# Windowed attention and two expert layers: the second expert's two products by Strassen's scheme

## The chip, the cores and the metric

The kernel runs on one core of one Trainium2 chip. The metric is the device time of one execution in microseconds, the median of several runs. A profiled execution was taken beside them; all rows below come from it. TensorE runs the matmuls (PE in the rows; its weight loads are PEld), VectorE is DVE, ScalarE is ACT, GpSimd is POOL, and SyncE (SP) issues most transfers; POOL issues those of the weights.

## What is computed

Comments on the right tell the sizes.

```python
def _attn_ref(q, k, v, mem_k, mem_v):          # 4 x 8 heads, 768 rows of 64
    ...
    for c in range(nc):                          # chunks of 32 rows, 16 to the left, 8 to the right, 8 memory rows
        ...
        scores = scale * np.matmul(q_c, k_full.transpose(0, 1, 3, 2))
        scores = scores - np.max(scores, axis=-1, keepdims=True)
        a = np.exp(scores)
        a = a / (np.sum(a, axis=-1, keepdims=True) + 1e-09)
        out[:, :, c_start:c_end] = np.matmul(a, v_full)

def _moe_ref(x, w_in, w_out):                    # 3072 x 512, 512 x 2048, 2048 x 512
    h = x @ w_in
    g = h * np.cos(h)
    return (g @ w_out).astype(np.float32)

def _moe2_ref(x, w1, w2, w3, w_out):             # 3072 x 512, three 512 x 768, 768 x 512
    h = np.maximum(np.maximum(x @ w1, x @ w2), x @ w3)
    return (h @ w_out).astype(np.float32)
```

All is float32. Both kernels split an operand of a large product into a rounded high part and the rest (the low part), and add three products: high by high, high by low, low by high.

## The kernel before

**Stage 1** works on eight blocks of 384 tokens (`BLK`), block t with the first expert while the attention of block t+1 is slipped in between. One step f of 16 makes 128 of the 2048 hidden columns (`hidden` on PE, 12 matmuls of 384 columns) and adds hidden column group f-3 (`second`, 12 matmuls of 384 columns) to the four banks of the result (`LAG` = 3). ACT scales and rounds the hidden values (L505, L507), DVE forms the remainder (L667), ACT takes sine and square (L514, L516), DVE multiplies and splits into `gh` and `gl` (L671, L677, L680). The result of a block goes to DRAM (`y_dram`).

**Stage 2** works on the same eight blocks. For one of six groups m of 128 hidden columns, PE makes three branches (12 matmuls of 384 columns each, `branch`), ACT copies the first from PSUM (L598), DVE takes the largest of the three (L755, L758) and splits it (L764, L766), and PE multiplies the group before by the output weights (`project`, L461 to L463, 9 matmuls of 512 columns, three banks of 128 tokens). A block is 6 x (36 + 9) matmuls.

**Weights** come in slots of 1024 columns a partition: POOL issues the load into `wraw` (two buffers), ACT rounds it (`high_w`, L535), POOL subtracts (`low_w`, L288). The ones of stage 2 take the place of stage 1's in `wts`, slot by slot, during the last block of stage 1, one a step from step 4 on: ACT's `high_w(NF + f - LAG - 1)` stands ahead of `hidden(t, f)` in its order.

**What sets the order**: no scheduler. Each engine has its own program, written by hand, and executes it strictly in that order; semaphores tie the engines together. An engine that waits holds up all that stands behind the wait in its own program. The two stages' middle blocks run in hardware loops (`Fori`).

The three lines that make every large product:

```python
pe.matmul(o, wh, mh, start=start, stop=False)          # L306
pe.matmul(o, wh, ml, start=False, stop=False)          # L307
return pe.matmul(o, wl, mh, start=False, stop=stop)    # L308
```

## Times and profile before

| | |
|---|---|
| median of 3 runs | 1063.84 us (1062.72 to 1064.02) |
| the profiled execution's own time | 1065.7 us |
| its span, first to last instruction | 1063.9 us |
| PE busy | 1028.1 us, 97% of the span |
| DVE, ACT, POOL busy | 493.2, 386.4, 83.7 us |
| stage 1 ends, by the last split of its hidden values | about 659 us |
| chain that ended last | PE 89%, ACT 4%, DVE 3%, DMA 3% |

Matmuls overlap: the 384-column ones take 0.33 us each but start every 0.173 us, so the distance between starts is what a matmul costs. A busy row is a duration; a row's last bracket tells how long the engine stood idle before it and for whom.

### The profile page before, as it was taken

To read this page: it belongs to the slowest core of one execution; us is meant where nothing else is said; L and a number is where in the kernel's file an instruction comes from. 1 tells how busy PE (TensorE), PEld (TensorE's weight loads), DVE (VectorE), ACT (ScalarE), POOL (GpSimd) and SP (SyncE) were. 2 spreads that over 40 slices of the span, in tenths; PEclk is the share of its full clock that TensorE was granted. 3 is DMA by queue.
4 is the path that set the end of the run, shared out by engine and by line. 5 is a ranking of instruction groups with operands and counts; after the bars stand their busy time and mean duration, and the time that the engine had idled before them with its cause. 6 is when DMAs were issued, how large, how long until landed. Compare 5 with 4: busy or idle time off the path is not lost.

```text
span 1063.9 us, 17509 instructions
## 1 busy us (share of the span) xinstructions
PE 1028.1 (97%) x6976; PEld 981.0 (92%) x6976; DVE 493.2 (46%) x876; ACT 386.4 (36%) x703; POOL 83.7 (8%) x64
## 2 busy tenths in 40 slices
PE   5789999999999999999999999999999999999998
PEld 4688999999999999999999988999999999999997
DVE  5477555554554555554655566323232223323222
ACT  2566454454454464464454554111010110101000
POOL 1555000000000000000000354000000000000000
PEclk7899999999999999999999999999999999999999
DMA  8754240231321321321311231201000000000000
GB/s 206 186 153 137 52 110 22 76 83 41 82 59 41 90 50 41 92 49 40 90 31 40 70 103 57 89 20 41 30 30 30 30 30 30 30 30 30 0 30 30
DMA packets 35712, 65.97 MB, mean 62 GB/s; under 512 B 2368, under 2 KB 26944, under 8 KB 35648
## 3 DMA queue, kind: packets, MB, share of 16 engines
q1 hardware_dynamic: 31616, 50.34, 17.3%
...
## 4 chain that ended last, share of the span: by engine, by line
PE 89%; ACT 4%; DVE 3%; DMA 3%; issue 2%; POOL 0%; SPq 0%; ACTq 0%; DVEq 0%
PE ps L306 25%; PE ps L308 24%; PE ps L307 24%; PE ps L462 3%; PE ps L463 3%; PE ps L461 3%; PE ps L351 2%; PE ps L325 2%; DVE stage_and_tiles L667 2%; DMA qk<-qk_in 1%; PE ps L359 1%; PE ps L338 1%; ACT wts L535 1%; DMA wraw<-w_in 1%; ACT stage_and_tiles L514 1%
## 5 line engine op out<-in xcount | busy, mean ns | idle before, releaser
L306 PE MATMUL ps<-xh,wts 128*128 128x384 f32 x1088 | 373.7, 344 | 3.5 <-issue 2.1
L308 PE MATMUL ps<-xh,wts 128*128 128x384 f32 x1088 | 365.5, 336 | 0.0
L307 PE MATMUL ps<-xl,wts 128*128 128x384 f32 x1088 | 364.7, 335 | 0.0
L306 PEld LDWEIGHTS ps<-xh,wts 128*128 128x128 f32 x1088 | 204.8, 188 | 14.9 <-issue 11.0
L667 DVE SCALAR_TENSOR_TENSOR stage_and_tiles<-stage_and_tiles 128x384 f32<-128x384 f32 x128 | 101.6, 794 | 240.5 <-ACT stage_and_tiles L507 240.5
L307 PEld LDWEIGHTS ps<-xl,wts 128*128 128x128 f32 x1088 | 205.0, 188 | 2.0
L308 PEld LDWEIGHTS ps<-xh,wts 128*128 128x128 f32 x1088 | 204.7, 188 | 0.0
L306 PE MATMUL ps<-gh,wts 128*128 128x384 f32 x512 | 171.9, 336 | 3.9 <-DVE gl L680 3.9
L308 PE MATMUL ps<-gh,wts 128*128 128x384 f32 x512 | 171.4, 335 | 0.0
L307 PE MATMUL ps<-gl,wts 128*128 128x384 f32 x512 | 171.1, 334 | 0.0
L598 ACT COPY stage_and_tiles<-ps 128x384 f32<-128x384 f32 x48 | 23.0, 479 | 306.0 <-PE ps L308 305.5
L505 ACT ACTIVATE stage_and_tiles<-ps 128x384 f32<-128x384 f32 x128 | 62.7, 490 | 162.2 <-PE ps L308 159.2
L755 DVE TENSOR_TENSOR stage_and_tiles<-stage_and_tiles,ps 128x384 f32<-128x384 f32 x48 | 26.6, 554 | 201.4 <-PE ps L308 201.4
L288 POOL TENSOR_TENSOR wts<-wraw,wts 128x1024 fp32r<-128x1024 f32 x28 | 66.8, 2384 | 550.9 <-ACT wts L535 550.9
L514 ACT ACTIVATE stage_and_tiles<-stage_and_tiles 128x384 f32<-128x384 f32 x128 | 67.2, 525 | 99.9 <-DVE stage_and_tiles L667 99.1
L306 PEld LDWEIGHTS ps<-gh,wts 128*128 128x128 f32 x512 | 96.1, 188 | 6.5 <-DVE gl L680 6.5
L307 PEld LDWEIGHTS ps<-gl,wts 128*128 128x128 f32 x512 | 96.1, 188 | 0.0
L308 PEld LDWEIGHTS ps<-gh,wts 128*128 128x128 f32 x512 | 96.1, 188 | 0.0
L680 DVE TENSOR_TENSOR gl<-stage_and_tiles,gh 128x384 fp32r<-128x384 f32 x128 | 71.5, 558 | 4.4
L507 ACT ACTIVATE stage_and_tiles<-ps,rounder 128x384 f32<-128x384 f32 x128 | 73.5, 574 | 0.0
L671 DVE SCALAR_TENSOR_TENSOR stage_and_tiles<-stage_and_tiles 128x384 f32<-128x384 f32 x128 | 70.4, 550 | 0.0
L516 ACT ACTIVATE stage_and_tiles<-stage_and_tiles 128x384 f32<-128x384 f32 x128 | 67.2, 525 | 4.0
...
## 6 DMA issues: line engine op xcount, KB each, us to landing
...
wraw<-w_in POOLq DMA_DIRECT2D x28, 512.0 KB, 3.7
...
y_dram<-stage_and_tiles SPq DMA_DIRECT2D x8, 768.0 KB, 6.5
qk<-y_dram SPq DMA_DIRECT2D x8, 768.0 KB, 4.3
out<-stage_and_tiles SPq DMA_DIRECT2D x8, 768.0 KB, 3.5
...
```

The costliest lines, as they stand in the source:

```text
L288: pool.tensor_tensor(wts[:, s, :, 1, :], wraw[:, g % 2, :, :], wts[:, s, :, 0, :].bitcast(F32), ALU.subtract).then_inc(w_ready, 1)
L306: pe.matmul(o, wh, mh, start=start, stop=False)
L307: pe.matmul(o, wh, ml, start=False, stop=False)
L308: return pe.matmul(o, wl, mh, start=False, stop=stop)
L461: pe.matmul(o, gh[:, m % 3, toks], w[:, 0, :], start=(m == 0), stop=False)
L505: act.activation(hid[:, f % 2, :], ps[:, HB[f % 2], 0:BLK], ACT.Copy, scale=1.0 / (2 * PI)).then_inc(h_copied, 1)
L507: act.activation(ang[:, f % 2, :], ps[:, HB[f % 2], 0:BLK], ACT.Identity, scale=1.0 / (2 * PI), bias=rounder[:, :]).then_inc(turns_done, 1)
L514: act.activation(a, a, ACT.Sin, scale=BELOW_PI).then_inc(sin_done, 1)
L516: act.activation(a, a, ACT.Square, scale=ROOT_TWO).then_inc(cos_done, 1)
L667: dve.scalar_tensor_tensor(out=a, in0=a, scalar=ROUND, in1=hid[:, f % 2, :], op0=ALU.subtract, op1=ALU.subtract).then_inc(r_done, 1)
L671: dve.scalar_tensor_tensor(out=hp, in0=ap, scalar=1.0, in1=hp, op0=ALU.subtract, op1=ALU.mult).then_inc(g_done, 1)
L680: dve.tensor_tensor(glp, hp, ghp.bitcast(F32), ALU.subtract).then_inc(g_ready, 1)
```

## The change

Stage 1 stays, but for the last block's extra work. **Stage 2** is done anew, on six blocks of 512 tokens (`BLK2`). A product of 2 x 2 blocks is made with seven block products in place of eight (the Winograd form of Strassen's scheme). Blocks of the input are 128 model columns by 256 tokens, blocks of the weights 128 by 128.

- A **unit** of the first product (54 of them: 6 blocks x 3 pairs of column groups x 3 branches) is seven products 1, 5, 7, 2, 6, 4, 3 of 6 matmuls with 256 columns: 42. A unit of the second product (12: 6 blocks x 2 halves) is seven products of 9 matmuls with 256 columns: 63. PE interleaves products 7 and 4 of unit n-1 with the other five of unit n. All in all 3024 matmuls of 256 columns; before there were 1728 of 384 and 432 of 512. Every product has its own wait, products 6, 3, 7 and 4 for a copy or sum of what lies in their bank, since they add onto it.
- ACT copies three banks of 256 columns a unit (`snap`, products 1, 5, 6), DVE adds four quarters (`c11`, `c12`, `c22`, `c21`) and takes the largest (`largest`, 768 columns).
- **Operands in seven forms.** Each weight unit (9 of the branches and 3 of the output weights) is loaded by POOL in two transfers, POOL makes four sums of 256 columns (`sums_rows`, `sums_columns`), ACT rounds 1792 columns (`high_w2`), POOL subtracts 1792 columns (`low_w2`). Two raw buffers. The input of each block gets four sums of 512 columns (DVE, `y_sums_of`) and seven roundings and subtractions of 512 columns (`high_y` on ACT, `y_low` on DVE).
- **The hidden values** of the second product go out to DRAM (`h2_dram`, 18 pieces, 512 KB each) and come back from the end of the first product on: SP loads, POOL sums (`sums_hidden`, 4 x 256 columns), ACT rounds (`high_h`, 1792 columns), DVE subtracts (`h_low`, 1792 columns). `H_STEPS` places the roundings in ACT's and DVE's program, from unit 50 on.
- All of stage 2 is written out without loops. Buffers are cut from three arenas (`arena_w`, `arena_a`, `arena_f`).

```diff
+HALF = 256
+BLK2 = 2 * HALF
+NBLK2 = B * S // BLK2
+NPAIR = NM // 2
+UNITS = NPAIR * NB2
+UNITS_A = NBLK2 * UNITS
+TAUS = HALF // SUB
+UNITS_ALL = UNITS_A + NBLK2 * TAUS
+HUNITS = NBLK2 * NPAIR
+UCOLS = 2 * 7 * HALF
+RAWCOLS = 7 * HALF
+RING = 9
+ORDER = (1, 5, 2, 6, 3, 7, 4)
+W_AT = {1: 0, 2: 1, 5: 2, 4: 3, 6: 4, 7: 5, 3: 6}
+W2B_AT = {1: 0, 7: 1, 2: 2, 3: 3, 5: 4, 6: 5, 4: 6}
+H_AT = {1: 0, 5: 1, 4: 2, 2: 3, 6: 4, 7: 5, 3: 6}
...
+        W2_STEPS = (5, 7, 9, 10, 12, 14)
+        H_STEPS = ((0,), (1,), (2,), (3,), (4, 5), (6,), (7, 8), (9,), (10, 11), (12,), (13, 14), (15,), (16, 17)) + ((),) * 6
...
+        BANK_A, BANK_B, BANK_C = (2, 1), (6, 7, 4), (5, 0)
...
+            for blk in range(NBLK2):
+                if blk < NBLK2 - 1:
+                    load_y(blk + 1)
+                else:
+                    load_h(0)
+                    load_h(1)
+                store_hidden2(3 * blk)
+                if blk == NBLK2 - 1:
+                    load_h(2)
+                store_hidden2(3 * blk + 1)
+                if blk == NBLK2 - 1:
+                    load_h(3)
+                store_hidden2(3 * blk + 2)
+            for r in range(4, 7):
+                load_h(r)
+            for blk in range(NBLK2):
+                for r in range(3 * blk + 7, min(3 * blk + 10, HUNITS)):
+                    load_h(r)
+                for tau in range(TAUS):
+                    store_out(TAUS * blk + tau)
...
+            def load_h(r):
+                sp.wait_ge(fours_stored[r % 2], 16 * (r // 2) + 16)
+                if r < 2:
+                    sp.wait_ge(y_ready, 7 * NBLK2)
+                elif r < 4:
+                    sp.wait_ge(w2_ready, UNITS + r)
+                else:
+                    sp.wait_ge(hm_ready, r - 3)
+                sp.dma_start(raw_h[r % 4][:, 0:4, :], h2_dram[r, :, :].rearrange("p (q c) -> p q c", q=4))\
+                  .then_inc(h_landed[r % 4], 16)
...
+            def load_w2(u):
+                if u == 0:
+                    pool.wait_ge(w_ready, NF)
+                elif u == 1:
+                    pool.wait_ge(pv_done, SUBS)
+                else:
+                    pool.wait_ge(w2_ready, u - 1)
...
+            def sums_rows(r, sums, base):
+                pool.tensor_tensor(r[:, 5, :], r[:, 0, :], r[:, 2, :], ALU.subtract).then_inc(sums, 1)
+                pool.tensor_tensor(r[:, 2, :], r[:, 2, :], r[:, 3, :], ALU.add).then_inc(sums, 1)
+                pool.wait_ge(sums, base + 2)
+                pool.tensor_tensor(r[:, 4, :], r[:, 2, :], r[:, 0, :], ALU.subtract).then_inc(sums, 1)
+                pool.wait_ge(sums, base + 3)
+                pool.tensor_tensor(r[:, 6, :], r[:, 1, :], r[:, 4, :], ALU.subtract).then_inc(sums, 1)
...
+            load_w2(0)
+            load_w2(1)
+            sums_w2(0)
+            for u in range(UNITS + NPAIR):
+                if u + 1 < UNITS + NPAIR:
+                    sums_w2(u + 1)
+                low_w2(u)
+                if u + 2 < UNITS + NPAIR:
+                    load_w2(u + 2)
+            for r in range(HUNITS):
+                pool.wait_ge(h_landed[r % 4], 16 * (r // 4) + 16)
+                sums_hidden(raw_h[r % 4], hm_sums, 4 * r)
...
+            def product6(n):
+                pe.wait_ge(s1_copied, n + 1)
+                product(n, 6, bank_b(n))
...
+            def product7(n):
+                pe.wait_ge(s6_copied, n + 1)
+                product(n, 7, bank_b(n))
+
+            def product4(n):
+                pe.wait_ge(c22_done, n + 1)
+                product(n, 4, bank_b(n))
+
+            for n in range(UNITS_ALL + 1):
+                if n < UNITS_ALL:
+                    product1(n)
+                    product5(n)
+                if n:
+                    product7(n - 1)
+                if n < UNITS_ALL:
+                    product2(n)
+                    product6(n)
+                if n:
+                    product4(n - 1)
+                if n < UNITS_ALL:
+                    product3(n)
...
+            def high_w2(u):
+                if u < UNITS:
+                    last = -(-UCOLS * (u + 1) // 2048) - 1
+                    act.wait_ge(y_done, NF * (NBLK - 1) + last + 1)
+                else:
+                    act.wait_ge(p_done[4], UNITS_A - UNITS + u - UNITS + 1)
+                act.wait_ge(w2_sums, 4 * u + 4)
+                act.copy(unit_w(u % UNITS)[:, 0, :, :], raw2[u % 2]).then_inc(w2_high, 1)
+
+            def high_h(r):
+                if r < 6:
+                    act.wait_ge(p_done[4], UNITS_A - UNITS + 3 + r + 1)
+                elif r < 8:
+                    act.wait_ge(p_done[4], UNITS_A)
+                else:
+                    act.wait_ge(p_done[4], UNITS_A + TAUS * ((r - 8) // NPAIR + 1))
+                act.wait_ge(hm_sums, 4 * r + 4)
+                act.copy(unit_h(r)[:, 0, :, :], raw_h[r % 4]).then_inc(hm_high, 1)
...
+                    if last and f in W2_STEPS:
+                        high_w2(W2_STEPS.index(f))
+                    if last and f in (11, 13, 15):
+                        high_y(0, (f - 11) // 2)
...
+            def snap(n, p, bank, s, spent, copied):
+                act.wait_ge(p_done[p], n + 1)
+                if n >= 2:
+                    act.wait_ge(spent, n - 1)
+                act.copy(snaps[:, n % 2, s, :], bank).then_inc(copied, 1)
...
+            for n in range(UNITS_ALL + 1):
+                blk, u = divmod(n, UNITS)
+                if n < UNITS_ALL:
+                    snap(n, 1, bank_b(n), 0, c11_done, s1_copied)
+                    snap(n, 5, bank_c(n), 1, c22_done, s5_copied)
+                if n < 3:
+                    high_w2(6 + n)
+                if n < UNITS_A:
+                    if blk < NBLK2 - 1 and u == 6:
+                        high_y(blk + 1, 0)
+                        high_y(blk + 1, 1)
+                    if blk < NBLK2 - 1 and u == 8:
+                        high_y(blk + 1, 2)
+                        high_y(blk + 1, 3)
+                    if blk and u == 0:
+                        high_y(blk, 4)
+                        high_y(blk, 5)
+                if n < UNITS_ALL:
+                    snap(n, 6, bank_b(n), 2, c12_done, s6_copied)
+                if blk and u == 0 and n < UNITS_A:
+                    high_y(blk, 6)
+                if n and (n > UNITS_A or (n - 1) % NB2 == 0):
+                    corner(n - 1)
+                if UNITS_A - 7 <= n < UNITS_A - 4:
+                    high_w2(UNITS + n - UNITS_A + 7)
+                if UNITS_A - 4 <= n:
+                    done = H_STEPS[n - UNITS_A + 4]
+                    for r in done:
+                        high_h(r)
...
+            def h_low(r):
+                dve.wait_ge(hm_high, r + 1)
+                dve.tensor_tensor(unit_h(r)[:, 1, :, :], raw_h[r % 4], unit_h(r)[:, 0, :, :].bitcast(F32),
+                                  ALU.subtract).then_inc(hm_ready, 1)
...
+            def c22(n):
+                dve.wait_ge(p_done[7], n + 1)
+                dve.wait_ge(s5_copied, n + 1)
+                dve.tensor_tensor(place(n, 2), snaps[:, n % 2, 1, :], bank_b(n), ALU.add).then_inc(c22_done, 1)
...
+            for n in range(UNITS_ALL + 1):
+                blk, u = divmod(n, UNITS)
+                before = n - 1
+                if n:
+                    c22(before)
+                    if before < UNITS_A and before % NB2:
+                        largest(before)
+                if blk and u == 0 and n < UNITS_A:
+                    y_low(blk, 4)
+                if n < UNITS_ALL:
+                    c11(n)
+                if n and before < UNITS_A and before % NB2:
+                    c21(before)
+                if blk and u == 0 and n < UNITS_A:
+                    y_low(blk, 5)
+                    y_low(blk, 6)
+                if n < UNITS_ALL:
+                    c12(n)
+                if n < UNITS_A:
+                    if blk < NBLK2 - 1 and u == 5:
+                        y_sums_of(blk + 1)
+                    if blk < NBLK2 - 1 and u == 6:
+                        y_low(blk + 1, 0)
+                        y_low(blk + 1, 1)
+                    if blk < NBLK2 - 1 and u == 8:
+                        y_low(blk + 1, 2)
+                        y_low(blk + 1, 3)
+                if UNITS_A - 4 <= n:
+                    for r in H_STEPS[n - UNITS_A + 4]:
+                        h_low(r)
```

**PE, in the middle of stage 2.** Before, the end of a `project` and the begin of a branch:

```order
L461 MATMUL ps<-wts,gh 128x512
L462 MATMUL ps<-wts,gh 128x512
L463 MATMUL ps<-wts,gl 128x512
L306 MATMUL ps<-xh,wts 128x384 [waits third_maxed]
L307 MATMUL ps<-xl,wts 128x384
L308 MATMUL ps<-xh,wts 128x384
```

After, the end of product 2 and the first half of product 6 of one unit:

```order
L474 MATMUL ps<-arena_a,arena_w 128x256
L472 MATMUL ps<-arena_a,arena_w 128x256 [waits s1_copied]
L473 MATMUL ps<-arena_a,arena_w 128x256
L474 MATMUL ps<-arena_a,arena_w 128x256
L472 MATMUL ps<-arena_a,arena_w 128x256
```

A wait stands ahead of every 6 matmuls (of 12 before), on ACT or DVE each time.

**POOL, the weights of stage 2.** Before, from one slot to the next:

```order
L288 TENSOR_TENSOR wts<-wraw,wts 128x2x512 [waits w_high]
L283 DMA wraw<-w_in 128x1024 [waits w_ready]
L288 TENSOR_TENSOR wts<-wraw,wts 128x2x512 [waits w_high]
L283 DMA wraw<-w_in 128x1024 [waits w_ready]
L288 TENSOR_TENSOR wts<-wraw,wts 128x2x512 [waits w_high]
```

After, from one unit to the next, and where the hidden values' sums begin:

```order
L451 TENSOR_TENSOR arena_w<-arena_f,arena_w 128x1792 [waits w2_high]
L416 DMA arena_f<-w_in 128x512 [waits w2_ready]
L416 DMA arena_f<-w_in 128x512
L429 TENSOR_TENSOR arena_f<-arena_f 128x256 [waits raw2_landed1]
L431 TENSOR_TENSOR arena_f<-arena_f 128x256 [waits w2_sums]
L432 TENSOR_TENSOR arena_f<-arena_f 128x256
L434 TENSOR_TENSOR arena_f<-arena_f 128x256 [waits w2_sums]
L451 TENSOR_TENSOR arena_w<-arena_f,arena_w 128x1792 [waits w2_high] x2
L437 TENSOR_TENSOR arena_f<-arena_f 128x256 [waits h_landed0]
```

The load of unit u+2 stands behind the subtraction of unit u, and its sums, which wait for the landing, stand ahead of the subtraction of unit u+1.

**ACT, units 49 to 51 of stage 2.** Before, the groups of the last block of stage 2:

```order
L598 COPY stage_and_tiles<-ps 128x384 [waits m_ready,br_done]
L581 COPY stage_and_tiles<-ps 128x512 [waits out_stored,o_done]
L581 COPY stage_and_tiles<-ps 128x512
L598 COPY stage_and_tiles<-ps 128x384 [waits m_ready,br_done] x5
L581 COPY stage_and_tiles<-ps 128x512 [waits out_stored,o_done]
```

After:

```order
L803 COPY arena_f<-ps 128x256 [waits c12_done,p6_done]
L812 COPY arena_f<-ps 128x256 [waits fours_stored0,p4_done]
L739 CAST arena_w<-arena_f 128x1792 [waits w2_sums,p4_done]
L803 COPY arena_f<-ps 128x256 [waits c11_done,p1_done]
L803 COPY arena_f<-ps 128x256 [waits c22_done,p5_done]
L803 COPY arena_f<-ps 128x256 [waits c12_done,p6_done]
L749 CAST arena_w<-arena_f 128x1792 [waits hm_sums,p4_done]
L803 COPY arena_f<-ps 128x256 [waits c11_done,p1_done]
```

The copy that product 6 of unit 51 waits for (last row) now stands behind two roundings that wait for POOL's sums.

## Rows read from the trace of the kernel before

**Rows 1.** The page's part 1: busy time, share of the span, instructions.

```profile
PE 1028.1 (97%) x6976; PEld 981.0 (92%) x6976; DVE 493.2 (46%) x876; ACT 386.4 (36%) x703; POOL 83.7 (8%) x64
```

**Rows 2.** Timeline of PE in stage 2: start us, us, engine, line, operation.

```profile
762.21 0.33 PE L308 MATMUL ps<-xh,wts 128*128 128x384 f32 x1
762.38 0.39 PE L461 MATMUL ps<-wts,gh 128*128 128x512 f32 x1
762.61 0.40 PE L462 MATMUL ps<-wts,gh 128*128 128x512 f32 x1
762.84 0.40 PE L463 MATMUL ps<-wts,gl 128*128 128x512 f32 x1
763.08 0.39 PE L461 MATMUL ps<-wts,gh 128*128 128x512 f32 x1
```

**Rows 3.** Timeline of ACT: the same group's copy, six groups apart.

```profile
674.95 0.48 ACT L598 COPY stage_and_tiles<-ps 128x384 f32<-128x384 f32 x1 [7.87 <-PE ps L308]
...
725.03 0.48 ACT L598 COPY stage_and_tiles<-ps 128x384 f32<-128x384 f32 x1 [7.87 <-PE ps L308]
```

**Rows 4.** Timeline of weight loads and matmuls, from four transposes back to `hidden`.

```profile
240.73 0.60 PE L338 MATMUL ps<-ident,prob 128*128 128x128 f32 x4
241.06 0.19 PEld L306 LDWEIGHTS ps<-xh,wts 128*128 128x128 f32 x1
241.08 0.42 PE L306 MATMUL ps<-xh,wts 128*128 128x384 f32 x1
241.17 0.19 PEld L307 LDWEIGHTS ps<-xl,wts 128*128 128x128 f32 x1
```

**Rows 5.** Timeline of POOL in the last block of stage 1.

```profile
602.49 2.40 POOL L288 TENSOR_TENSOR wts<-wraw,wts 128x1024 fp32r<-128x1024 f32 x1 [1.69 <-ACT wts L535]
605.18 0.57 POOL L283 DMA_DIRECT2D wraw<-w_in  x1 [0.30 <-POOL wts L288]
```

**Rows 6.** The page's part 6: KB each, us from issue to landing.

```profile
wraw<-w_in POOLq DMA_DIRECT2D x28, 512.0 KB, 3.7
qk<-y_dram SPq DMA_DIRECT2D x8, 768.0 KB, 4.3
```

**Rows 7.** Groups by line and shape: count, busy us, mean ns of one, idle before.

```profile
L535 ACT CAST wts<-wraw 128x1024 fp32r<-128x1024 f32 x28 | 29.0, 1034 | 1.9 <-DMA wraw<-w_in 1.9
L526 ACT CAST xh<-qk 128x1536 fp32r<-128x1536 f32 x8 | 11.9, 1482 | 0.0
L581 ACT COPY stage_and_tiles<-ps 128x512 f32<-128x512 f32 x16 | 8.6, 590 | 48.2 <-PE ps L463 48.2
L758 DVE TENSOR_TENSOR stage_and_tiles<-stage_and_tiles,ps 128x384 f32<-128x384 f32 x48 | 26.6, 554 | 71.1 <-PE ps L308 71.1
```

**Rows 8.** Timeline of ACT in the last block of stage 1, its step 3.

```profile
593.84 0.49 ACT L505 ACTIVATE stage_and_tiles<-ps 128x384 f32<-128x384 f32 x1 [0.73 <-PE ps L308]
594.23 0.57 ACT L507 ACTIVATE stage_and_tiles<-ps,rounder 128x384 f32<-128x384 f32 x1
```

**Rows 9.** DVE: L667's durations (smallest/median/largest, ns); L690's group as in Rows 7.

```profile
L667 DVE SCALAR_TENSOR_TENSOR stage_and_tiles<-stage_and_tiles x128: 495/558/2016, 39.5 to 654.5; 128x384 f32<-128x384 f32 x128
L690 DVE TENSOR_TENSOR xl<-qk,xh 128x1536 fp32r<-128x1536 f32 x8 | 15.0, 1869 | 2.0 <-ACT xh L526 2.0
```

**Rows 10.** Stretches at the start: busy time of each engine, PEclk the granted clock.

```profile
5.50:9.00 3.50, 0.00 (x0) 0.00 (x0) 1.82 (x2) 0.00 (x0) 0.00 (x0) 0.90 1.05 234
9.00:15.70 6.70, 4.77 (x68) 3.73 (x68) 2.36 (x5) 0.63 (x1) 0.52 (x1) 0.50 1.11 226
34.00:38.00 4.00, 3.71 (x12) 3.70 (x12) 0.24 (x1) 1.51 (x2) 3.13 (x3) 0.50 0.23 46
38.00:42.00 4.00, 4.00 (x47) 3.34 (x46) 2.37 (x3) 3.40 (x6) 2.76 (x2) 0.87 0.57 161
42.00:47.00 5.00, 2.16 (x13) 1.84 (x11) 3.21 (x4) 2.92 (x6) 2.93 (x2) 1.00 0.97 248
```

**Rows 11.** Timeline of ACT at the end of the kernel.

```profile
1058.83 1.07 ACT L581 COPY stage_and_tiles<-ps 128x512 f32<-128x512 f32 x2 [7.80 <-PE ps L463]
```

461 lines of the change are left out of this document (274 added, 187 removed).

## The prediction, made before the change was run

> **What bounds the kernel now.** I read part 1 first: PE is busy 97% of the span [rows 1], so a gain has to come from fewer or shorter matmuls, and every wait of PE costs its full length. Next the timeline of PE in stage 2 [rows 2]: matmuls follow each other without a gap, 0.17 us from start to start at 384 columns, 0.70 us for three at 512. ACT's copy of the same group comes back 50.08 us later after one block [rows 3], which is 216 matmuls of 384 and 54 of 512 columns. With 0.2333 us for a 512 (0.70 / 3), a 384 takes (50.08 - 54 x 0.2333) / 216 = 0.1735 us. Eight blocks are 400.6 us. PE's last matmul ends at 1058.8 [rows 11], so stage 2 has an equivalent start at 1058.8 - 400.6 = 658.2 us. I compare the new kernel with this number: its equivalent start plus its matmuls plus its waits.
>
> **Part 1, the matmuls: a gain.** Columns fall from 8 x (216 x 384 + 54 x 512) = 884,736 to 3024 x 256 = 774,144, by an eighth, but there are 3024 matmuls instead of 2160. So the price of a 256-column matmul decides, which no row shows. Three readings. A straight line through 0.1735 at 384 and 0.2333 at 512 gives 0.1137. The same time per column as at 384 gives 0.1157. The 13.5 ns that a 384 takes over its 160 ns at 2.4 GHz (384 / 2.4), taken as a fixed price, gives 0.1067 + 0.0135 = 0.1202. And a floor: behind the transposes, which are short, the weight load of L306 starts at 241.06, its matmul waits for it (0.42 us instead of 0.33), and the next load, which elsewhere starts together with the matmul before it, starts at 241.17 [rows 4]. A weight load thus holds a matmul back by 0.11 us, so a 256 costs no less than 0.11. I take 0.1155, since two of the readings lie beside it, and keep 0.11 and 0.1202. 3024 x 0.1155 = 349.3 us, a gain of 51.3 (37.1 with 0.1202; 68.0 with 0.11).
>
> The row says that a 384 takes 13.5 ns over its columns. The Trainium skill (TensorE: Matmul & The Clock Gate, Back-to-back issue gap) gives the columns at 2.4 GHz plus 2.5 ns, 109 ns for 256 columns; 3024 of them would be 330 us, 20 less than my term. The same page (LDWEIGHTS) puts a weight load of 128 columns at 107 ns; by this the trace agrees (0.11), and it speaks against shrinking a matmul to 256 columns, because nothing is left under which the load hides.
>
> **Part 2, the weights' preparation at the end of stage 1: a loss.** Follow POOL's order: subtract unit u, issue the load of u+2, wait for it, four sums, subtract unit u+1. Nothing overlaps, since the load needs the buffer that the subtraction frees. One round: subtraction 2.40 x 1792 / 1024 = 4.2; a gap of 0.3 and two issues of 0.57, of which the second's landing counts: 0.3 + 0.57 + 3.7 = 4.6 [rows 5, 6]; four sums of a quarter of 2.40 each and two hand-overs of 0.3: 3.0. Together 11.8 us. The transfer is of half the size of the row's, so 3.0 is possible, and the sums could be nearly free of hand-overs: 10.5 at the low end; DVE's own operations in POOL's way (below) and dearer small sums make 13 at the high end.
> When does it begin? ACT's first such rounding stands behind its step 5 of the last block. Step 3 starts at 593.84 [rows 8]; two steps of 24 matmuls are 2 x 24 x 0.1735 = 8.3, the two scalings some 1.0, the rounding of 1792 columns 1.71 (1034 ns for 1024, 1482 for 1536 [rows 7], so 0.875 ns a column). POOL's first subtraction starts at 593.8 + 8.3 + 1.0 + 1.7 = 604.8. The sums of unit 8 are there seven rounds later, 687.4. ACT stands before them in its program between the copies of products 5 and 6 of unit 2, so the copy of product 6 ends at 687.4 + 1.7 + 0.4 = 689.5 (256 columns from PSUM: 590 ns for 512 [rows 7], 0.37 by the same slope), and only then can product 7 of unit 2 start. PE has done 21 products of 6 matmuls by then, 14.6 us, so the equivalent start is 674.9: **+16.7 us** (from +7 to +25 by the two ends of the round). It takes the form of two idle stretches of PE, of 6 to 7 us each, in units 2 and 3. The stalls that PE has in the last block of stage 1 before, and those it has after, vanish in this, since POOL's chain is longer than both.
>
> **Part 3, the turn from the first product to the second: a loss.** Units now last 42 x 0.1155 = 4.85 us, later 63 x 0.1155 = 7.28. Count from the start of unit 47. ACT rounds unit 9 of the weights until 5.8 (behind product 6 and its copy). POOL: subtraction to 10.0, load and sums of unit 11 to 17.6, two subtractions to 26.0, sums of hidden piece 0 to 29.0. ACT waits for these behind unit 50, rounds until 30.7 and copies product 1 of unit 51 until 31.1. Product 6 of unit 51, which waits for that copy, was due at 4 x 4.85 + 4 x 0.693 = 22.2: 8.9 us late. DVE then subtracts piece 0 for about 2.05 us (1869 ns for 1536 columns [rows 9], and 0.42 for the sum behind it), which makes product 4 another 1.3 late: 10.2.
> The second place: SP issues the loads of pieces 4 and 5 behind the store of piece 17, and this waits for `c21` of unit 53, 6.2 us into unit 54. Landing 4.0 later (512 KB: 3.7, 768 KB: 4.3 [rows 6]) plus 0.4 of SP, two times 3.0 of POOL's sums, 1.7 of rounding, 0.4 of copy: 18.7. ACT waits through all of it, ahead of the copy of product 1 of unit 55. Product 6 of unit 55 was due at 6.6 + 4.2 = 10.7: 8.0 late, and 1.1 more for `c22` behind DVE's subtraction: 9.1. Together **+19.3 us**. With sums at 2.0 and landings a microsecond shorter it is 13; with sums at 3.6, longer landings and DVE in POOL's way, 25. Pieces 6 to 17 come in time by the same reckoning: a unit of 7.28 us holds 1.5 roundings and subtractions, 1.5 x (3.0, 1.7, 2.05) on POOL, ACT, DVE.
>
> **Part 4, smaller terms.** DVE's four sums of 512 columns of the next input (some 0.7 us each by L758 [rows 7]) stand ahead of `c22` once in each of five blocks: it ends about 0.65 us after product 4 was due, and `y_low` makes product 3 some 0.15 late: **+4** (0 to 8). The clock: with no matmul from 5.5 to 9.0 us the granted clock in the next stretch is 0.50, and under dense work from 34 to 38 it is still 0.50, then 0.87; a gap of 3 us within 42 to 47 leaves it at 1.00 [rows 10]. So idle stretches of 6 to 9 us should drop it to 1.2 GHz, and it comes back after some 4 us of work; at 256 / 1.2 = 213 ns a matmul that costs 4 x (1 - 0.1155 / 0.213) = 1.8 us. Four stretches; the first hides in POOL's chain, the others partly behind `c22`: **+4.5** (0 to 9). The end: product 4 of the last unit waits for `c22` of product 7, +0.8, while the copies and stores behind it are smaller than the 512-column ones [rows 11]: **+0.5**. At nothing I put the copies, quarter sums and `largest` of a unit in the steady part: ACT's 3 x 0.37 and DVE's 3 x 0.42 + 0.9 fit into 4.85 us, and each wait has two or more products between (1.39 us for `c22`, which needs 0.42 and the 0.16 by which a matmul's record outlasts the next one's start [rows 2]). Uncovered, each would cost its excess 54 times; POOL is idle there.
> A DVE operation with two SBUF inputs takes 2.0 us instead of 0.558 where it meets POOL [rows 9]; `largest`, `y_low` and `h_low` are of this kind, and it is why Parts 2 and 3 have high ends.
>
> **The sum.** Span 1063.9 - 51.3 + 16.7 + 19.3 + 4 + 4.5 + 0.5 = 1057.6. The profiled execution took 1065.7 with this span, 1.9 above the median of 1063.84, so the timed median should be about 1057.6 + 1.8 - 1.9 = 1057.5; I say 1058.
>
> **Rivals.**
> - *A 256 costs the fixed 13.5 ns* (0.1202): 14.2 us more, **1072**, slower. For it: 13.5 ns is what 384 shows, and the first of the three 512s (762.38 to 762.61) is near 213 + 13.5 too. Against: the others are longer. It decides from 0.1155 + 8.5 / 3024 = 0.1183 us on; from there the kernel is slower.
> - *A 256 runs near the floor* (0.11): 16.6 us less, **1041**. Against it: no large matmul in the trace comes within 8% of its columns' time.
> - *Preparation is cheaper*, small sums and landings at the low ends: 9 less in Part 2, 6 in Part 3, **1042**.
> - *Preparation is dearer*, POOL and DVE hold each other up in both places, the clock stays low longer: **1078**.
> That the change doesn't do what it says is excluded: the order has the 3024 matmuls.
>
> **Chances.** Forecast 38% (1050 to 1068), fixed price 27%, floor 6%, cheaper preparation 14%, dearer 15%. A measurement of this kernel can tell about 0.2%, 2.1 us. Faster by more (below 1061.7): 24 of the forecast's 38, 3 of the fixed price's 27, all 6, 13 of 14: 46%. Same: 8 + 3 + 1 = 12%. Slower: 6 + 21 + 0 + 15 = 42%. Range 1038 to 1082; the forecast's own is 1050 to 1068.
>
> **What would show it.** The start-to-start time of the 256-column matmuls, 0.1155 us; POOL's round of 11.8 us from 604.8 on, and PE idle twice for 6 to 7 us between 670 and 690; PE idle for 7 to 9 us twice around units 51 and 55, both ended by ACT's copy, ACT's rounding ended by POOL; the granted clock at 0.50 after each. I am wrong if the time per matmul is off, if PE does not stop at these places, or if it stops every unit in the steady part.

## The result, and the profile after

The changed kernel is slower: 1076.12 us median of 4 runs (1073.15 to 1076.43) against 1063.28 (1062.33 to 1064.02) before, a ratio of 1.0115 with a 95% interval of 1.0095 to 1.0135. The forecast was 1058. What came is the first rival: a matmul of 256 columns takes 0.120 us, and the rest is where it was expected.

The page of the kernel after, part 1, parts of parts 5 and 6 (columns as in [rows 1], [rows 7] and [rows 6]):

```profile
span 1074.3 us, 20000 instructions
PE 1007.9 (94%) x7840; PEld 977.1 (91%) x7840; DVE 591.5 (55%) x1022; ACT 486.2 (45%) x919; POOL 218.0 (20%) x196
...
L451 POOL TENSOR_TENSOR arena_w<-arena_f,arena_w 128x1792 fp32r<-128x1792 f32 x12 | 50.0, 4173 | 235.6 <-ACT arena_w L739 235.6
...
arena_f<-w_in POOLq DMA_DIRECT2D x24, 256.0 KB, 3.1
```

PE is busy for 94% of a longer span, against 97% [rows 1]. It idles more, and it also has more to do than I thought. The timeline of PE in the middle of stage 2 answers to [rows 2]: every start is 0.12 us behind the one before.

```profile
899.75 0.28 PE L472 MATMUL ps<-arena_a,arena_w 128*128 128x256 f32 x1
899.87 0.28 PE L473 MATMUL ps<-arena_a,arena_w 128*128 128x256 f32 x1
899.99 0.28 PE L474 MATMUL ps<-arena_a,arena_w 128*128 128x256 f32 x1
```

Over the whole stage the median distance is 120 ns, and so are its tenth and ninetieth percentiles. The 3024 matmuls take 362.9 us.

The four idle stretches, in the timeline of PE (the last bracket is the idle time and who ended it; smaller ones are left out):

```profile
679.56 0.58 PE L472 MATMUL ps<-arena_a,arena_w 128*128 128x256 f32 x1 [4.51 <-ACT arena_f L803]
...
690.45 0.39 PE L472 MATMUL ps<-arena_a,arena_w 128*128 128x256 f32 x1 [3.58 <-ACT arena_f L803]
...
946.61 0.58 PE L472 MATMUL ps<-arena_a,arena_w 128*128 128x256 f32 x1 [6.35 <-ACT arena_f L803]
...
984.76 0.58 PE L472 MATMUL ps<-arena_w 128*128 128x256 f32 x1 [10.38 <-ACT arena_f L803]
```

They stand where they were forecast, ahead of product 7 of units 1 and 2 and of product 6 of units 51 and 55, and ACT's copy (`snap`, L803) ends each. Why that copy is late, the timeline of ACT shows: it stands behind a rounding of 1792 columns that waited for POOL's sums, in the last place behind two of them.

```profile
688.44 1.69 ACT L739 CAST arena_w<-arena_f 128x1792 fp32r<-128x1792 f32 x1 [8.11 <-POOL arena_f L426]
690.03 0.92 ACT L803 COPY arena_f<-ps 128x256 f32<-128x256 f32 x3
...
944.60 1.69 ACT L749 CAST arena_w<-arena_f 128x1792 fp32r<-128x1792 f32 x1 [8.25 <-POOL arena_f L442]
946.19 0.64 ACT L803 COPY arena_f<-ps 128x256 f32<-128x256 f32 x2
...
978.12 1.69 ACT L749 CAST arena_w<-arena_f 128x1792 fp32r<-128x1792 f32 x1 [9.44 <-POOL arena_f L442]
...
982.75 1.69 ACT L749 CAST arena_w<-arena_f 128x1792 fp32r<-128x1792 f32 x1 [2.94 <-POOL arena_f L442]
984.35 0.64 ACT L803 COPY arena_f<-ps 128x256 f32<-128x256 f32 x2
```

And POOL's round of preparation in its timeline, undisturbed by DVE: subtraction, two issues, wait for the landing, four sums.

```profile
677.42 4.00 POOL L451 TENSOR_TENSOR arena_w<-arena_f,arena_w 128x1792 fp32r<-128x1792 f32 x1
681.72 1.09 POOL L416 DMA_DIRECT2D arena_f<-w_in  x2 [0.30 <-POOL arena_w L451]
685.32 0.73 POOL L421 TENSOR_TENSOR arena_f<-arena_f 128x256 f32<-128x256 f32 x1 [2.51 <-DMA arena_f<-w_in]
...
687.63 0.72 POOL L426 TENSOR_TENSOR arena_f<-arena_f 128x256 f32<-128x256 f32 x1
688.31 4.00 POOL L451 TENSOR_TENSOR arena_w<-arena_f,arena_w 128x1792 fp32r<-128x1792 f32 x1
```

That is 10.9 us. The first subtraction started at 603.5 and the eighth at 688.3, so seven rounds took 12.1 us each on average.

The stretches of the clock (columns as in [rows 10]):

```profile
684.00:691.00 7.00, 3.42 (x27) 3.21 (x27) 0.84 (x2) 2.51 (x4) 5.52 (x5) 0.99 0.08 33
691.00:694.40 3.40, 3.40 (x18) 3.40 (x17) 1.71 (x3) 0.11 (x1) 2.41 (x3) 0.50 0.12 39
694.40:700.00 5.60, 5.60 (x49) 5.60 (x48) 1.69 (x4) 1.38 (x4) 3.52 (x5) 1.00 0.44 168
...
943.60:953.80 10.20, 6.51 (x28) 6.22 (x29) 6.25 (x7) 4.66 (x6) 8.87 (x10) 0.50 0.20 65
...
977.70:991.30 13.60, 6.48 (x28) 6.19 (x29) 5.15 (x4) 6.16 (x7) 13.13 (x15) 0.50 0.28 97
```

Behind the last three of the four stretches the clock is granted at 0.50, 1.2 GHz, for 18, 28 and 28 matmuls. With 0.213 us instead of 0.12 these are 1.7, 2.6 and 2.6 us. Behind the stretch of unit 1 it is at 0.50 as well, until 684; that lies ahead of the second wait for POOL's chain.

### The profile page after: what moved, and what is told of

Its sections match the earlier page's. It is cut to its first block, busy times and chain, and to the rows that moved or that the text cites. A ratio compares the mean times of both kernels' runs of the same rounds, so it can differ in the third digit from the quotient of the medians.

```text
span 1074.3 us, 20000 instructions
## 1 busy us (share of the span) xinstructions
PE 1007.9 (94%) x7840; PEld 977.1 (91%) x7840; DVE 591.5 (55%) x1022; ACT 486.2 (45%) x919; POOL 218.0 (20%) x196
## 4 chain that ended last, share of the span: by engine, by line
PE 79%; POOL 8%; DMA 6%; issue 2%; ACT 2%; DVE 2%; SPq 0%; ACTq 0%; DVEq 0%
PE ps L472 25%; PE ps L474 24%; PE ps L473 24%; POOL arena_w L451 4%; DMA arena_f<-w_in 3%; PE ps L517 2%; PE ps L491 2%; DMA arena_f<-qk_in 1%; PE ps L525 1%; PE ps L504 1%; DVE arena_f L907 1%; POOL arena_f L422 1%; POOL arena_f L421 1%; POOL arena_f L424 1%; POOL arena_f L426 1%
## 5 line engine op out<-in xcount | busy, mean ns | idle before, releaser
L472 PE MATMUL ps<-arena_a,arena_w 128*128 128x384 f32 (+1 forms) x1780 | 573.1, 322 | 29.3 <-ACT arena_f L803 15.7
L474 PE MATMUL ps<-arena_a,arena_w 128*128 128x384 f32 (+1 forms) x1780 | 562.3, 316 | 0.0
L473 PE MATMUL ps<-arena_a,arena_w 128*128 128x384 f32 (+1 forms) x1780 | 561.8, 316 | 0.0
L472 PEld LDWEIGHTS ps<-arena_a,arena_w 128*128 128x128 f32 x1780 | 342.6, 192 | 42.7 <-ACT arena_f L803 16.6
L473 PEld LDWEIGHTS ps<-arena_a,arena_w 128*128 128x128 f32 x1780 | 342.8, 193 | 0.0
L474 PEld LDWEIGHTS ps<-arena_a,arena_w 128*128 128x128 f32 x1780 | 342.3, 192 | 0.0
L907 DVE SCALAR_TENSOR_TENSOR arena_f<-arena_f 128x384 f32<-128x384 f32 x128 | 92.7, 725 | 240.1 <-ACT arena_f L698 240.1
L803 ACT COPY arena_f<-ps 128x256 f32<-128x256 f32 x198 | 72.8, 374 | 206.9 <-PE ps L474 206.9
L696 ACT ACTIVATE arena_f<-ps 128x384 f32<-128x384 f32 x128 | 62.8, 490 | 169.7 <-PE ps L474 159.4
L705 ACT ACTIVATE arena_f<-arena_f 128x384 f32<-128x384 f32 x128 | 67.3, 526 | 84.4 <-DVE arena_f L907 83.9
L451 POOL TENSOR_TENSOR arena_w<-arena_f,arena_w 128x1792 fp32r<-128x1792 f32 x12 | 50.0, 4173 | 235.6 <-ACT arena_w L739 235.6
L920 DVE TENSOR_TENSOR arena_a<-arena_f,arena_a 128x384 fp32r<-128x384 f32 x128 | 73.6, 575 | 4.4
L698 ACT ACTIVATE arena_f<-ps,rounder 128x384 f32<-128x384 f32 x128 | 73.6, 575 | 0.0
L911 DVE SCALAR_TENSOR_TENSOR arena_f<-arena_f 128x384 f32<-128x384 f32 x128 | 72.8, 568 | 0.0
L1026 DVE TENSOR_TENSOR arena_f<-arena_f,ps 128x256 f32<-128x256 f32 x66 | 27.7, 420 | 80.4 <-PE ps L474 66.6
L707 ACT ACTIVATE arena_f<-arena_f 128x384 f32<-128x384 f32 x128 | 67.2, 525 | 4.1
L472 PE MATMUL ps<-arena_w 128*128 128x256 f32 x196 | 57.4, 293 | 10.4 <-ACT arena_f L803 10.4
L1006 DVE TENSOR_TENSOR arena_f<-arena_f,ps 128x256 f32<-128x256 f32 x66 | 27.7, 419 | 68.1 <-PE ps L474 68.1
L473 PE MATMUL ps<-arena_w 128*128 128x256 f32 x196 | 56.7, 289 | 0.0
L474 PE MATMUL ps<-arena_w 128*128 128x256 f32 x196 | 56.6, 289 | 0.0
```

The source lines that it names most:

```text
L451: pool.tensor_tensor(w[:, 1, :, :], raw2[u % 2], w[:, 0, :, :].bitcast(F32), ALU.subtract)\
L472: pe.matmul(o, wh, mh, start=start, stop=False, skip_group_check=onto)
L473: pe.matmul(o, wh, ml, start=False, stop=False, skip_group_check=onto)
L474: return pe.matmul(o, wl, mh, start=False, stop=stop, skip_group_check=onto)
L696: act.activation(hid[:, f % 2, :], ps[:, HB[f % 2], 0:BLK], ACT.Copy, scale=1.0 / (2 * PI)).then_inc(h_copied, 1)
L698: act.activation(ang[:, f % 2, :], ps[:, HB[f % 2], 0:BLK], ACT.Identity, scale=1.0 / (2 * PI), bias=rounder[:, :]).then_inc(turns_done, 1)
```

## The experiments

| kernel | median us (runs) | ratio, 95% interval | span, us | PE idle, half clock in stage 2, us |
|---|---|---|---|---|
| before | 1063.28 to 1063.56 | | 1063.9 | |
| after | 1076.12 (4) | 1.0115, 1.0095 to 1.0135 | 1074.3 | 32.6, 10.3 |
| a_late78 | 1066.31 (10) | 1.0023, 1.0009 to 1.0036 | 1065.6 | 26.4, 7.3 |
| a_turn | 1059.48 (5) | 0.9952, 0.9936 to 0.9969 | 1060.2 | 20.2, 7.6 |
| a_both | 1049.65 (4) | 0.9872, 0.9850 to 0.9894 | 1045.7 | 12.9, 3.3 |
| a_both2 | 1047.71 (5) | 0.9850, 0.9837 to 0.9864 | 1045.6 | 11.3, 4.9 |
| a_fill | 1074.93 (4) | 1.0098, 1.0079 to 1.0118 | 1074.9 | 14.5 and 22.8 of filler, 5.1 |
| a_spfirst | 1066.38 (1) | | 1064.6 | 25.0, 7.9 |
| a_sums8 | 1057.39 (1) | | 1055.6 | 23.9, 6.6 |

The last column sorts the distances between starts of stage 2's matmuls: over 0.26 us the excess is idle time, over 0.13 it is put down to the half clock; the rest is 3024 x 0.12 = 362.9. For after the three sum up to 405.8, against 405.7 us from its first start, 664.8, to its last end, 1070.5. (Of its 10.3, 7.9 lie where the granted clock is 0.50; the rest are short waits.) The spans are those of one profiled execution each, and the last two kernels were run only once.

### p_widths: what a matmul costs at each width

Before plus series of 48 matmuls at PE's end, whose results nobody uses:

```diff
+            def series(cols, wide, moving, stationary, bank, count=48, step=128):
+                for i in range(count):
+                    at = (i * step) % 1024
+                    pe.matmul(ps[0:wide, bank + i // 6 % 2, 0:cols], stationary[:, at:at + wide],
+                              moving[:, 1024:1024 + cols], start=True, stop=True)
+            for cols in (128, 192, 256, 320, 384, 448, 512):
+                series(cols, 128, flat_w, flat_x, 4)
+            for cols in (256, 384):
+                for wide in (96, 64, 32):
+                    series(cols, wide, flat_w, flat_x, 4)
+            series(256, 128, flat_x, flat_w, 4)
+            series(256, 128, flat_w, flat_x, 4, step=0)
```

> The kernel before, with series of 48 matmuls each added behind the last product on TensorE (results thrown away): 128, 192, 256, 320, 384, 448 and 512 columns with a weight load of 128 columns; then 256 and 384 columns with weight loads of 96, 64 and 32 columns; then 256 columns with the operands' places swapped, and with one and the same weights each time. Read: the time from start to start. Theory 'a fixed price beside every matmul': 128 columns at the weight load's 0.11 us, 192 at 0.11, 256 at 0.120, 320 at 0.147, 384 at 0.1735, 448 at 0.200, 512 at 0.227. Theory 'more time per column': 256 at 0.116, 320 at 0.145, 448 at 0.202. If the price comes from the weight load that runs beside the matmul, it shrinks with the load: 13 ns at 128 columns of weights, some 3 at 32 (256 columns at 0.110). If it belongs to the matmul itself, 256 columns stay at 0.120 with every width.

Rows of its timeline of PE. A row of n matmuls gives the distance as (length - duration of one) / (n - 1), with durations of 0.274, 0.283, 0.334, 0.368, 0.390 us and, for the last, 0.276:

```profile
1059.80 0.72 PE L484 MATMUL ps<-wts,xh 128*128 128x128 f32 x5
1069.79 0.76 PE L484 MATMUL ps<-wts,xh 128*128 128x256 f32 x5
1084.73 0.85 PE L484 MATMUL ps<-wts,xh 128*128 128x384 f32 x4
1093.78 0.78 PE L484 MATMUL ps<-wts,xh 128*128 128x448 f32 x3
1103.73 0.84 PE L484 MATMUL ps<-wts,xh 128*128 128x512 f32 x3
...
1117.82 0.73 PE L484 MATMUL ps<-wts,xh 128*64 128x256 f32 x5
```

Over the whole series, medians of the distances in ns:

| columns | 128 | 192 | 256 | 320 | 384 | 448 | 512 |
|---|---|---|---|---|---|---|---|
| measured | 111 | 111 | 120 | 147 | 173 | 207 | 227 |
| columns / 2.4 + 13.5 | 66.8 | 93.5 | 120.2 | 146.8 | 173.5 | 200.2 | 226.8 |

So the price is fixed, 13.5 ns a matmul, from 256 to 512 columns (but for 448, 7 ns more), and at 192 columns and below a floor of 111 holds. With weights 96, 64 and 32 wide a 384 stays at 173 or 174: there the weight load has no part in the price. A 256 falls to 116, 113 and 113, though: 6.3 of its 13.5 ns remain. Two more series of 256 columns, one with the operands' places swapped and one with the same weights each time, stayed at 120. The fixed price of the rival and the floor from [rows 4] are thus parts of one curve. With the 0.227 and 0.173 of these series a straight line through 512 and 384 gives 0.119 at 256 columns; mine took 0.70 / 3 = 0.2333 for a 512.

The Trainium skill (TensorE: Matmul & The Clock Gate, Back-to-back issue gap) adds 2.5 ns to the columns' time for the gap of an isolated matmul; for a stream of weight loads and matmuls it gives about 81 ns at 128 columns and 131 at 512. Neither fits here: the runs have 13.5 ns over the columns at four widths, 111 ns at 128 columns and 227 at 512.

### a_late78: Part 2's mechanism

ACT's roundings of weight units 7 and 8 later in its program, at units 3 and 5 of stage 2, not 1 and 2:

```diff
-                if n < 3:
-                    high_w2(6 + n)
+                if n in (0, 3, 5):
+                    high_w2({0: 6, 3: 7, 5: 8}[n])
```

> The changed kernel with ScalarE's roundings of weight units 7 and 8 moved from units 1 and 2 to units 3 and 5 of its program; nothing else. My theory of Part 2 (ScalarE waits for GpSimd's sums ahead of the copy that product 7 needs): both idle stretches of TensorE at 675 and 687 us go (4.8 + 3.9 us and what the fall of the clock cost there, about 2), so 10 to 12 us less than the changed kernel, and no new wait up to unit 9, since unit 8's weights are ready about 703 us and unit 8 starts after 705. Rival, that the weights themselves come too late (unit 7 or 8 waits for w2_ready instead): gain under 4 us and a new wait at unit 7 or 8.

It gained 9.8 us, and both stretches at 675 and 687 are gone; 2.7, 1.0 and 0.5 us remain at 698, 708 and 719. Only the 1.0 us at 708 is a wait for the weights themselves (for POOL's L451), so their preparation was hardly too slow for PE. ACT reached it too early in its program and waited there with the copies behind it.

### a_turn and a_spfirst: Part 3's mechanism

a_turn moves the sums of hidden pieces 0 and 1 between those of the output weights on POOL, and lets SP issue the loads of pieces 4 and 5 ahead of the store of piece 17. ACT rounds pieces 0 and 1 one unit earlier and weight unit 11 one unit later, each where its sums are ready; DVE's subtractions of pieces 0 to 2 move with them. The core of it:

```diff
             for u in range(UNITS + NPAIR):
+                if u == UNITS + 1:
+                    sums_h(1)
                 if u + 1 < UNITS + NPAIR:
                     sums_w2(u + 1)
+                if u == UNITS:
+                    sums_h(0)
                 low_w2(u)
...
                     load_h(3)
+                    load_h(4)
+                    load_h(5)
                 store_hidden2(3 * blk + 2)
...
-        H_STEPS = ((0,), (1,), (2,), (3,), (4, 5), (6,),
+        H_STEPS = ((0,), (1,), (), (2,), (3,), (4, 5), (6,),
...
-                if UNITS_A - 4 <= n:
-                    done = H_STEPS[n - UNITS_A + 4]
+                if UNITS_A - 5 <= n:
+                    done = H_STEPS[n - UNITS_A + 5]
```

> The changed kernel with the turn to the second product in another order, the same work: GpSimd sums hidden pieces 0 and 1 ahead of the last weight units, SyncE issues pieces 4 and 5 ahead of the store of piece 17, ScalarE rounds unit 11 of the weights and each piece where its data is there. My theory of Part 3: the idle stretches at 933, 940, 948 and 974 us (19.5 us together) shrink to 0 to 4, and the time at half clock behind them (about 9 us lost) goes too: 22 to 28 us less than the changed kernel. Rival, that the second product waits for DRAM or for VectorE's subtractions whatever the order: 5 to 12 us less, the wait moves to unit 54 or 56.

It gained 16.6 us, less than the 22 to 28 expected. The stretches of 6.6 and 10.7 us are gone, but a new one of 5.3 stands at 941, and 2.6 us in two pieces from 970 on. The new one comes from POOL and DVE holding each other up, seen best in a_both below.

a_spfirst has of this only SP's two lines.

> The changed kernel with one thing moved: SyncE issues the loads of hidden pieces 4 and 5 ahead of the store of piece 17. My theory of the second place of Part 3: the idle stretch of 10.7 us at 974 shrinks to 0 to 2 and the half clock behind it goes (about 6 us): 13 to 17 us less; the first place (6.6 us around unit 51) stays as it is. Rival, that the landings or GpSimd's sums set the end there: under 5 us less.

The span fell by 9.7 us. The 10.7 us ahead of product 6 of unit 55 are gone and the stretch of unit 51 stayed, as the view of PE's waits of stage 2 shows (total us, times, longest), the first two rows of after, the second two of a_spfirst:

```profile
PE ps L472 <- ACT arena_f L803: 26.1, 5, 10.4
PE ps L472 <- DVE arena_f L1006: 2.1, 3, 0.9
```

```profile
PE ps L474 <- ACT arena_f L805: 17.5, 4, 6.4
PE ps L474 <- DVE arena_f L1008: 3.7, 6, 1.3
```

So the second stretch had its cause in SP's queue: the loads stood behind a store that waited for the last results of the block. POOL's sums were ready to take them. It gave less than the 13 to 17 us expected. I had put 6 us of half clock behind that stretch, where 2.6 are; the waits for DVE grew by 1.6 us; and the stretches of units 1 and 2, which this edit doesn't touch, were 1.4 us longer in this one execution.

### a_both and a_both2: do the two add, and what is next

Both edits together.

> Both reorderings together. If the two losses are separate, the gains add: 33 to 40 us less than the changed kernel, about 1038 us, 2.4% faster than the kernel before. If a matmul of 256 columns at 0.120 us is all that then stands against the change, TensorE needs 362.9 us of matmuls from about 665 us on and the span is 1033 to 1037 us.

1049.65 us: 26.5 below after, against 9.8 + 16.6 = 26.4. The two gains add, but to less than the 33 to 40 expected. Of what is left the largest stretch is 5.0 us idle (5.3 by the distance between starts), ended by DVE's `c22` (L1017 here). DVE's and POOL's timelines at this place:

```profile
921.11 4.53 DVE L1042 TENSOR_TENSOR arena_f<-arena_f 128x768 f32<-128x768 f32 x1
...
926.23 5.15 DVE L956 TENSOR_TENSOR arena_w<-arena_f,arena_w 128x1792 fp32r<-128x1792 f32 x1
...
931.63 0.41 DVE L1017 TENSOR_TENSOR arena_f<-arena_f,ps 128x256 f32<-128x256 f32 x1
```

```profile
920.75 8.74 POOL L453 TENSOR_TENSOR arena_w<-arena_f,arena_w 128x1792 fp32r<-128x1792 f32 x2
929.46 2.51 POOL L439 TENSOR_TENSOR arena_f<-arena_f 128x256 f32<-128x256 f32 x1
```

POOL runs two subtractions of some 4.4 us in a row. `largest` (L1042) starts during the first, and ends 0.5 us behind the middle of the pair; `h_low` (L956, 2.02 where POOL leaves it alone) starts during the second and ends 1.9 us behind it; and POOL's next sum, 0.74 elsewhere, takes 2.51 while DVE's runs. In both directions one operation stands still until the other has ended. `c22`, which reads PSUM, takes its 0.41 throughout, but stands behind them in DVE's program. This agrees with the Trainium skill (SBUF — State Buffer, SBUF: two separate sides), by which a DVE operation with two SBUF inputs and a POOL operation that reads SBUF exclude each other for whole instructions; [rows 9] had the same in its longest duration.

a_both2 breaks up POOL's pair: the third output unit's sums come between the subtractions, its rounding one unit later.

```diff
                 if u == UNITS + 1:
                     sums_h(1)
+                elif u == UNITS + 2:
+                    sums_w2(u)
-                if u + 1 < UNITS + NPAIR:
+                if u + 1 < UNITS + NPAIR and u != UNITS + 1:
                     sums_w2(u + 1)
...
-                if n == UNITS_A - 4:
+                if n == UNITS_A - 3:
                     high_w2(UNITS + 2)
```

> Both reorderings, and GpSimd subtracts unit 10 of the weights before it sums unit 11, so that its two subtractions of 4.4 us don't lie end to end; ScalarE rounds unit 11 one unit later. In the version before, VectorE's 768-column maximum took 4.53 us instead of 0.87 and its 1792-column subtraction 5.15 instead of 2.02 while GpSimd was at these two, and TensorE stood idle for 5.3 us. If that is the cause, the stretch at 927 us shrinks to under 2 us and the half clock behind it goes: 4 to 6 us less than with both reorderings, 1043 to 1046 us. Rival, that VectorE meets the next of GpSimd's operations instead: no gain, the same stretch elsewhere.

The gap at 927 is gone (`h_low` at 923.84 took 2.55 us), but a new one of 3.4 us stands at 937, and POOL's last subtraction, met by `h_low`, took 5.48. The span is the same, the median 2 us lower; the intervals of the two ratios overlap. The rival came: DVE and POOL have this work to do within the same 30 us, and this shift moved the collision. At 1047.71 us this version beats the kernel before by 1.5%.

### a_fill: what the clock costs

The kernel after, with 34, 28, 48 and 80 matmuls of 256 columns into an unused bank, standing where PE waits in the four stretches. They compute nothing that is used.

```diff
...
+            def filler(count):
+                w = unit_w(0)
+                for _ in range(count):
+                    pe.matmul(ps[:, 3, 0:HALF], w[:, 0, 0, 0:P], w[:, 0, 1, :], start=True, stop=True)
...
                 if n:
+                    filler(FILL7.get(n - 1, 0))
                     product7(n - 1)
                 if n < UNITS_ALL:
                     product2(n)
+                    filler(FILL6.get(n, 0))
                     product6(n)
```

> The changed kernel with matmuls of 256 columns into an unused PSUM bank (results thrown away) put into the four idle stretches of TensorE: 34 ahead of product 7 of unit 1, 28 ahead of product 7 of unit 2, 48 ahead of product 6 of unit 51, 80 ahead of product 6 of unit 55. Each fills 80 to 90% of its stretch, so the waits themselves end when they did. Theory (half clock behind the stretches costs 11 us, the last two most of it): the granted clock stays at 1.00 there and the time falls by 7 to 11 us. Rival (the clock's share is hidden behind the same chains of waits): within 3 us of the changed kernel.

The stretches of the clock of a_fill, as above: 1.00 throughout around 690, and 1.00 instead of 0.50 from 978 to 985, but not to the end of the last place.

```profile
684.00:691.00 7.00, 5.80 (x49) 5.60 (x47) 0.63 (x2) 0.20 (x1) 3.63 (x6) 1.00 0.23 77
691.00:694.40 3.40, 1.59 (x13) 1.59 (x14) 0.96 (x3) 2.30 (x4) 3.40 (x1) 1.00 0.00 0
978.00:985.00 7.00, 6.16 (x52) 5.95 (x50) 2.29 (x1) 2.83 (x2) 6.76 (x8) 1.00 0.17 55
985.00:992.00 7.00, 5.11 (x29) 4.91 (x29) 2.91 (x3) 2.92 (x6) 6.69 (x8) 0.76 0.37 130
```

The half clock's share fell by half, from 10.3 to 5.1 us. But stage 2's matmuls still took 405.3 us from first start to last end, against 405.7, and the timed ratio is 0.0017 lower with intervals that overlap.

Part of this was lost ahead of the fillers. In this execution POOL's first subtraction started at 604.9, not 603.5, and its sums of unit 8 were done 2.4 us later, so product 7 of unit 2 started at 692.81 instead of 690.45. From there to the end of the last matmul it is 378.4 us against 380.1, with 3.4 us of half clock less: half of it came back. The rest, and the 1.9 us of half clock behind the stretch of unit 1, would then lie beside work that PE would have waited for. Behind product 6 of unit 55 comes product 4 of unit 54, which started 2.34 us later in after (987.10 behind 984.76) and 2.35 later in a_fill. It waits for `c22` in both, and DVE's subtraction stands ahead of that, as fast with a slow PE as with a fast one. Not settled is how much the clock costs in the kernel itself: 5.1 us of half clock remain in a_fill, and 1.7 us is no more than two executions of one kernel differ by.

### a_sums8: POOL's round shorter

The four sums of every branch weight unit are made of 8 columns a partition instead of 256; the rest of these sums is left out, nothing else is.

```diff
-                pool.tensor_tensor(r[:, 5, :], r[:, 0, :], r[:, 2, :], ALU.subtract).then_inc(sums, 1)
+                pool.tensor_tensor(r[:, 5, 0:8], r[:, 0, 0:8], r[:, 2, 0:8], ALU.subtract).then_inc(sums, 1)
...
```

> The changed kernel with GpSimd's four sums of each branch weight unit cut from 256 columns to 8 (so those weights are not formed; the part left out is the sums). Theory that GpSimd's round of 11.8 to 12.2 us sets the end of stage 1: the round falls to 9 us, the idle stretches at 675 and 687 go, and TensorE's waits in the last block of stage 1 fall from 10 us to under 4; 13 to 20 us less than the changed kernel. Rival, that the landing of the weights or ScalarE's order sets it: a round over 11 us and under 8 us less.

One round in POOL's timeline:

```profile
641.85 4.02 POOL L451 TENSOR_TENSOR arena_w<-arena_f,arena_w 128x1792 fp32r<-128x1792 f32 x1
646.17 1.10 POOL L416 DMA_DIRECT2D arena_f<-w_in  x2 [0.30 <-POOL arena_w L451]
649.87 0.20 POOL L421 TENSOR_TENSOR arena_f<-arena_f 128x8 f32<-128x8 f32 x1 [2.60 <-DMA arena_f<-w_in]
...
651.37 4.00 POOL L451 TENSOR_TENSOR arena_w<-arena_f,arena_w 128x1792 fp32r<-128x1792 f32 x1
```

A round is 9.5 us here, and the span fell by 18.7. Stage 2's first matmul starts at 658.5 instead of 664.8, the stretches at 675 and 687 are gone, and the last block of stage 1 loses 4.5 us less (9.6 against 14.1 by the distances between starts). Its waits alone are 7.0 us against 9.1; I had expected under 4. The turn kept its two (6.6 and 10.3). Product 7 of unit 2 starts at 673.7, which is an equivalent start of 658.6, next to the 658.2 of the kernel before. So all of Part 2's loss hangs on POOL's round.

## Why the prediction was wrong

Its sum, term by term, against the profiled execution of after. A measured term is the excess of the distances between starts over 0.12 us in its stretch.

| term | predicted | measured |
|---|---|---|
| equivalent start of stage 2 | 674.9 | 690.45 - 126 x 0.12 = 675.3 |
| Part 1, 3024 matmuls | 349.3 | 362.9 |
| Part 3, idle in the turn | 19.3 | 19.5 |
| Part 4, sums of the input | 4 | 3.1 |
| Part 4, clock | 4.5 | 1.7 + 2 x 2.6 = 6.9 |
| small waits in the turn and after it | 0 | 2.0 |
| end: last wait, and what follows the last matmul | 5.6 | 0.7 + 3.9 |
| span | 1057.6 | 1074.3 |

**The step that failed is Part 1's choice of 0.1155.** It is 13.6 of the 16.7 us. The measured time of a 256 is 0.120 us, in this kernel and in p_widths. The rows had the answer: a 384 takes 13.5 ns over its columns. I let two readings outvote that one. The same time per column rested on no mechanism. The straight line rested on 0.2333 for a 512, and more rows would not have mended it: over all of stage 2 before, a 512 takes 0.231 us on average and a 384 takes 0.174, and the line through these gives 0.117. Only series of one width each show 0.227, and with it 0.119. Why a 512 takes 4 ns more in the kernel, no run shows. One argument against the rivals was misread as well: that no large matmul comes within 8% of its columns' time. The first 512 of each three takes 0.228 us (median), 7% over the 0.2133 of its columns.

The rival's own condition decided as written: from 0.1183 us on the kernel is slower, and its 1072 is 4 us from the median. Of these, 2.5 are the smaller terms of the table. The other 1.9 is the step from span to median: the profiled execution before stood 1.9 above its median, the one after at its median. By the time of the columns alone the scheme saves an eighth, 46 us. Its 864 additional matmuls cost 11.7 of them at 13.5 ns each.

**Part 2 held**, to 0.4 us in part by luck: POOL began 1.3 us earlier than I said and its rounds were longer. Round 12.1 us on average (11.8), first subtraction at 603.5 (604.8), sums of unit 8 done at 688.3 (687.4), product 7 of unit 2 at 690.45 (689.5). The two stretches were 4.8 and 3.9 us long, not 6 to 7: more of the loss sits in stage 1's last block, where the distances between PE's starts exceed 0.173 us by 14.1 us, 9.1 of them waits and the rest mostly half clock (0.50 from 656.9 to 663.7). I had said that those stalls vanish in POOL's chain, and in the sum they do. a_late78 and a_sums8 show the mechanism from two sides. The round's parts came out differently: sums of 0.73 us instead of 0.6, transfers of 3.1 instead of 3.7, and DVE in the way in the rounds of stage 1, 11.7 to 12.7 us where an undisturbed one is 10.9. The one from 664.2 took 13.3, because POOL waited 4.8 us for the landing instead of 2.5.

**Part 3 held in size**, 19.5 us for 19.3, though the closeness of the sum is in part luck: 9.0 for 10.2 at unit 51 and 10.5 for 9.1 at unit 55. It held in mechanism: a_spfirst takes away the second place alone, a_turn both. The second is longer since `h_low` and POOL's sum met at 979.84 and 980.28. DVE's and POOL's timelines:

```profile
979.84 2.24 DVE L945 TENSOR_TENSOR arena_w<-arena_f,arena_w 128x1792 fp32r<-128x1792 f32 x1 [9.31 <-ACT arena_w L749]
```

```profile
975.03 0.72 POOL L437 TENSOR_TENSOR arena_f<-arena_f 128x256 f32<-128x256 f32 x1 [16.27 <-DMA arena_f<-h_dram]
...
980.28 2.38 POOL L442 TENSOR_TENSOR arena_f<-arena_f 128x256 f32<-128x256 f32 x1
```

What Part 3 left out shows only in the experiments: once the two waits are gone, POOL and DVE exclude each other for 5 us at the same place.

**Part 4.** The sums of the input cost 0.44 us in each of four blocks (0.17 in unit 6, 0.27 in unit 0 of the next) and 1.4 in the first: 3.1 in all where I had put 4. The first block's share was higher because DVE met POOL, which was making sums of weights. DVE's and POOL's timelines there:

```profile
706.98 0.69 DVE L933 TENSOR_TENSOR arena_f<-arena_f 128x512 f32<-128x512 f32 x1
707.59 1.23 DVE L934 TENSOR_TENSOR arena_f<-arena_f 128x512 f32<-128x512 f32 x1
708.85 1.11 DVE L936 TENSOR_TENSOR arena_f<-arena_f 128x512 f32<-128x512 f32 x1
```

```profile
708.35 1.06 POOL L431 TENSOR_TENSOR arena_f<-arena_f 128x256 f32<-128x256 f32 x1
```

The clock was mis-sized: I took one recovery of 4 us for every stretch, 18 matmuls, and it was 28 behind the two of the turn. But a_fill shows that such an account overstates it: of 3.4 us of half clock taken away behind unit 2, 1.7 came back, and the timed runs show no gain clear of their noise. The reservation in the prediction, that it hides partly behind `c22`, fits this run. The 2.0 us that I had not foreseen are the first matmul after each wait, which holds the next back by some 0.2 us more, and waits below 0.4. The end is 1.0 shorter than I took it: 3.7 us follow the end of the last matmul against 5.1 before (the table's 3.9 counts from 0.12 us behind its start), since a copy and store of 256 columns follow it, not of 512.

**The steady part** costs nothing, as predicted: outside the nine places of 0.17 and 0.27 just named the distances from 711 to 930 us are 0.12 on average, though every product has a wait of its own.
